# Both MLPs of a transform kernel as Strassen products, with weight combinations streamed from HBM

## The reference

```python
# attention without softmax, normalised per head
kv = einsum('bhsd,bhse->bhde', k, v); out = einsum('bhsd,bhde->bhse', q, kv)
x = out / sqrt(mean(out * out, -1) + 1e-6) * g_norm          # -> [B, S, D]
# first MLP: real part of a 2D Fourier transform, layer norm, MLP, residual
u = x + real(fft(fft(x, axis=1), axis=2))
x2 = u + relu(layer_norm(u) @ w_ch1) @ w_ch2                 # 512 -> 2048 -> 512
# second MLP: low-rank mixing over the tokens (rank 32), MLP, residual
u2 = x2 + transpose(transpose(x2) @ U @ V)
out = u2 + relu(u2 @ w_ch1b) @ w_ch2b
```

## Time and profile before

| what | value |
|---|---|
| median of 3 runs | 1966.59 us |
| the profiled execution, first to last instruction | 1964.7 us |
| granted TensorE clock, mean | 0.992 |
| TensorE busy | 1905.0 us, 97% |
| VectorE busy | 640.9 us, 33% |
| ScalarE busy | 359.1 us, 18% |
| GpSimd busy | 140.6 us, 7% |
| DMA | 94.96 MB, 48 GB/s over the span |

### The profile page before, as it was taken

The page is one execution under the profiler, slowest core; times in us unless marked ns, Lnnn a source line. Parts: engine busy times, 40 slices in busy tenths (PEclk is TensorE's granted clock), DMA queues, the critical chain, the costliest instruction groups (busy, mean ns, idle before and its releaser), DMA issues.

```text
span 1964.7 us, 24175 instructions
## 1 busy us (share of the span) xinstructions
PE 1905.0 (97%) x9764; PEld 1677.6 (85%) x9764; DVE 640.9 (33%) x1126; ACT 359.1 (18%) x784; POOL 140.6 (7%) x124
## 2 busy tenths in 40 slices
PE   5988799999999999999999999999999999999999
PEld 4777589999999999999988888888988888888988
DVE  4899962222222222222224321221222221221221
ACT  1333331111111111111123211211111111211111
POOL 1566530000000000000000000000000000000000
PEclk8999899999999999999999999999999999999999
DMA  8445230000000000000213100010000000000000
GB/s 298 163 157 168 95 120 33 1 32 32 31 1 32 32 0 32 32 32 0 80 58 107 65 33 17 17 34 7 27 33 1 33 33 17 17 17 1 17 17 16
DMA packets 23138, 94.96 MB, mean 48 GB/s; under 512 B 4833, under 2 KB 7265, under 8 KB 20130
## 3 DMA queue, kind: packets, MB, share of 16 engines
q1 hardware_dynamic: 23074, 94.01, 14.0%
HBM read 65.69 MB, written 28.31 MB: 48 GB/s over the span
## 4 chain that ended last, share of the span: by engine, by line
PE 88%; DVE 6%; DMA 1%; issue 1%; SPq 1%; POOL 1%; DVEq 0%; ACT 0%; POOLq 0%
PE bank L476 14%; PE bank L478 14%; PE bank L463 14%; PE bank L462 14%; PE bank L464 14%; PE bank L477 14%; PE bank L454 2%; DVE eo_sb L817 1%; DVE eo_sb L815 1%; DMA q_sb<-q_t 1%; PE bank L531 1%; POOL x_sb L1038 1%; DVE ss_sb L790 1%; SPq L209 1%; DVE x_sb L803 0%
## 5 line engine op out<-in xcount | busy, mean ns | idle before, releaser
L891 DVE SCALAR_TENSOR_TENSOR h_lo<-bank,h_hi 128x384 fp32r<-128x384 f32 x384 | 214.0, 557 | 1212.5 <-ACT h_hi L699 1212.5
L464 PE MATMUL bank<-at_hi,w_lo 128*128 128x384 f32 x1536 | 514.7, 335 | 2.1 <-issue 2.1
L462 PE MATMUL bank<-at_hi,w_hi 128*128 128x384 f32 x1536 | 515.0, 335 | 1.3 <-issue 1.3
L463 PE MATMUL bank<-at_lo,w_hi 128*128 128x384 f32 x1536 | 515.9, 336 | 0.0
L476 PE MATMUL bank<-w_hi,h_hi 128*128 128x512 f32 x1152 | 463.7, 403 | 0.0
L478 PE MATMUL bank<-w_hi,h_lo 128*128 128x512 f32 x1152 | 456.0, 396 | 0.0
L477 PE MATMUL bank<-w_lo,h_hi 128*128 128x512 f32 x1152 | 453.9, 394 | 0.0
L699 ACT ACTIVATE h_hi<-bank 128x384 fp32r<-128x384 f32 x384 | 189.2, 493 | 1369.2 <-PE bank L464 1369.2
L462 PEld LDWEIGHTS bank<-at_hi,w_hi 128*128 128x128 f32 x1536 | 288.4, 188 | 17.3 <-issue 2.1
L463 PEld LDWEIGHTS bank<-at_lo,w_hi 128*128 128x128 f32 x1536 | 288.1, 188 | 15.0
L464 PEld LDWEIGHTS bank<-at_hi,w_lo 128*128 128x128 f32 x1536 | 288.4, 188 | 2.7 <-issue 2.7
(11 more groups left out here) (84 smaller groups left out, 970.3 us busy)
## 6 DMA issues: line engine op xcount, KB each, us to landing
q_sb<-q_t SPq DMA_DIRECT2D x8, 1152.0 KB, 5.2
u_dram<-x_sb SPq DMA_DIRECT2D x24, 384.0 KB, 3.1
u_sb<-u_dram SPq DMA_DIRECT2D x12, 768.0 KB, 4.2
x_dram<-u_sb SPq DMA_DIRECT2D x12, 768.0 KB, 3.3
x_sb<-x_dram SPq DMA_DIRECT2D x12, 768.0 KB, 5.1
out<-u_sb SPq DMA_DIRECT2D x12, 768.0 KB, 3.3
k_sb<-k_main SPq DMA_DIRECT2D x7, 1024.0 KB, 5.2
v_sb<-v_main SPq DMA_DIRECT2D x7, 1024.0 KB, 7.6
```

The lines of the kernel that those rows point to most:

```text
L462: nc.tensor.matmul(ps[:, 0:TILE], w1_hi4[:, f, d, :], at_hi[:, d, :], start=(d == 0), stop=False)
L463: nc.tensor.matmul(ps[:, 0:TILE], w1_hi4[:, f, d, :], at_lo[:, d, :], start=False, stop=False)
L464: last = nc.tensor.matmul(ps[:, 0:TILE], w1_lo4[:, f, d, :], at_hi[:, d, :], start=False, stop=(d == ND - 1))
L891: nc.vector.scalar_tensor_tensor(h_lo[:, f % 2, :], hid_ps[f % 2][:, 0:TILE], 0.0, h_hi[:, f % 2, :].bitcast(F32), ALU.max, ALU.subtract). ...
```

## The change

**Strassen.** Both tiles of a pair are taken together: a group is 768 tokens of one MLP, and there are 12 groups (NG), six for each MLP (NS = 6). Each matrix product of a group is cut into 2 x 2 blocks and made as seven block products: activations `SIDE[i]` (a block, or the sum or difference of two) times a combination i of weight blocks. The seven results are added and subtracted into four blocks, partly in PSUM (products 2, 4 and 7 accumulate on each other in one bank pair, 5, 3 and 6 in another), partly by VectorE and ACT as they are read. Each product is still three matmuls of high and low parts. A step is (product i, block k) with 12 matmuls of 384 columns; a group has 28 up steps and 28 down steps. Both layers now give transposed outputs, so the first MLP's output is turned back by 144 transposes (`turn_out`), and the kernel's output is stored transposed.

```diff
-SPLIT_AT, GATHER_AT, TURN_AT, MIX_AT = 2, 3, 11, 12
+UP_STEPS = ([(1, k) for k in range(4)]
+            + [(i, 2 * h + j) for h in range(2) for i in (2, 4, 7) for j in range(2)]
+            + [(i, 2 * h + j) for h in range(2) for i in (5, 3, 6) for j in range(2)])
+DN_ORDER = (2, 5, 1, 4, 3, 7, 6)
+DN_STEPS = [(i, k) for i in DN_ORDER for k in range(4)]
+RING = 7
+ENT_RING = 5
+SIDE = {1: ("11", "22", 1), 2: ("11",), 3: ("12", "22", -1), 4: ("21", "11", -1), 5: ("22",), 6: ("11", "12", 1),
+        7: ("21", "22", 1)}
+OUT_AT = [1 + 4 * j for j in range(NCH)]
+POOL_KS = (3,)
...
+            def up_step(g, i, k):
+                e = UP_ENTRIES.index(i)
+                if k == 0:
+                    pe.wait_ge(lo_ready, entry(g, e))
+                w = weights_there(g, UP_SLOTS.index((i, k // 2)))
+                up_room(g, i, k)
...
+                for f in range(2):
+                    ps = pair[n][:, 512 * f:512 * f + TILE]
+                    for x in range(2):
...
+                        nc.tensor.matmul(ps, w_hi, hi[:, x, :], start=(fresh and x == 0), stop=False, skip_group_check=True)
+                        nc.tensor.matmul(ps, w_hi, lo[:, x, :], start=False, stop=False, skip_group_check=True)
+                        last = nc.tensor.matmul(ps, w_lo, hi[:, x, :], start=False, stop=(x == 1), skip_group_check=True)
```

```diff
+            def load_unit(unit):
+                name, n = unit[:2]
+                if n:
+                    sp.wait_ge(p_stored[name], 16 * n)
...
+            def store_unit(unit):
+                name, n, mlp, layer, f, x = unit
+                sp.wait_ge(p_lo[name], n + 1)
...
             next_kv(2)
-            sp.dma_start(w1_raw[:, :], w1a).then_inc(w_loaded[0][0], 16)
-            with sp.Fori(2, B - 1) as b:
+            load_unit(UNITS[1])
+            for b in range(2, B):
                 next_q(b)
-                next_kv(b + 1)
+                if b < B - 1:
+                    next_kv(b + 1)
+                store_unit(UNITS[b - 2])
+                load_unit(UNITS[b])
                 store_u(b - 2)
+            store_unit(UNITS[6])
+            load_unit(UNITS[8])
...
+            for q in range(NCH):
+                load_in(q)
...
+            store_unit(UNITS[7])
+            load_unit(UNITS[9])
+            store_unit(UNITS[8])
+            store_u(B - 2)
+            for n in range(RING):
+                load_w(n)
+            store_u(B - 1)
+            store_unit(UNITS[9])
...
+                        if t == 0:
+                            load_unit(UNITS[11])
+                            sp.wait_ge(last_stored, 16 * NT)
+                            load_unit(UNITS[10])
+                        if t in STORED_AT:
+                            store_unit(UNITS[10 + STORED_AT.index(t)])
...
             for g in range(NT):
                 weigh(0, g)
-            with pool.Fori(1, B) as b:
+            for b in range(1, B):
                 for g in range(NT):
                     weigh(b, g)
+                sum_unit(UNITS[b - 1])
                 for t in range(NT):
                     add_transform(b - 1, t)
```

More of the change, by code:

```diff
@@ L41, in build_program, with by_pool @@
+OUT_AT = [1 + 4 * j for j in range(NCH)]
+GATHER_AT = [4 + 4 * j for j in range(NCH)]
+MIX_AT = [28, 31, 34, 37, 41, 45]
+IN_AT = [30, 33, 36, 39, 43, 47]
+LN_AT = [8, 16, 38]
+STORED_AT = (4, 6, 12, 14, 20, 22)
+POOL_KS = (3,)
+def by_pool(i, k):
+    return k in POOL_KS
+def build_program(nc, k_main, k_rest, v_main, v_rest, q_t, g_norm, wr1a, wr2a, wr1b, wr2b, u_perm, v_perm,
+                  c_seq, s_seq, c_feat, s_feat, eye, u_dram, x2_dram, wc, out):
     F32 = mybir.dt.float32
@@ new lines, in build_program, with unit_blocks, raw_weights @@
+        UNIT_AT = {7 * (g - 1) + n: (g, 8 * n) for g in range(1, 6) for n in range(7) if 7 * (g - 1) + n < 32}
+        HALF_UNITS = {(g, n0): UNITS[16 + u] for u, (g, n0) in UNIT_AT.items()}
+        def unit_blocks(unit):
+            name, _, _, _, _, x = unit
+            _, raw, two = PB[name]
+            n = 1 if x is not None else 2
+            return [raw[:, n * i:n * (i + 1), 1, :] for i in range(7)], [two[:, i, :].rearrange("p (x c) -> p x c", x=n) for i in range(2)]
+        def raw_weights(unit, blk):
+            _, _, mlp, layer, f, x = unit
+            w = wr[mlp][layer][f]
+            return w[:, blk, :, :] if x is None else w[:, blk, x:x + 1, :]
@@ new lines, in gather @@
+            def gather(g, j):
+                n = NCH * g + j
+                tile, c = 2 * g + j // CH, j % CH
+                u = 3 * (tile % 3) + c
+                first, last = u == 0, u == 8
+                if n == 0:
+                    pe.wait_ge(up_split_lo, 1)
+                if first and n:
+                    pe.wait_ge(gt_lo_ready, tile // 3)
+                pe.wait_ge(x2_lo_ready, n + 1)
+                nc.tensor.matmul(gt_ps[0:64, :], up_hi[:, u, :], x2_hi[:, :], start=first, stop=False)
+                nc.tensor.matmul(gt_ps[0:64, :], up_lo[:, u, :], x2_hi[:, :], start=False, stop=False)
+                nc.tensor.matmul(gt_ps[0:64, :], up_hi[:, u, :], x2_lo[:, :], start=False, stop=last).then_inc(gathered, 1)
@@ L1052, in _, with raw_dn, add_first @@
+            def raw_dn(g, n):
+                i, k = DN_STEPS[n]
+                if len(SIDE[i]) > 1 and by_pool(i, k):
+                    raw(g, len(UP_ENTRIES) + n)
+            def add_first(g, block):
+                pool.wait_ge(dve_read, dve_count(g, "d1"))
+                nc.gpsimd.tensor_tensor(a_block(g, block), a_block(g, block), ch_block("22"), ALU.add).then_inc(v_ready, 1)
             for g in range(NT):
                 weigh(0, g)
-            with pool.Fori(1, B) as b:
+            for b in range(1, B):
@@ new lines, in _ @@
+            add_transform(B - 1, 0)
+            raw(0, 0)
+            add_transform(B - 1, 1)
+            add_transform(B - 1, 2)
+            sum_unit(UNITS[9])
+            raw(0, 2)
+            raw(0, 3)
+            for g in range(NG):
+                more = g < NG - 1
+                for t in range(NSTEP):
+                    if g == 0 and t + 2 in STORED_AT:
+                        sum_unit(UNITS[10 + STORED_AT.index(t + 2)])
+                    if t == 5:
+                        raw(g, 5)
+                    if t == 12:
+                        raw(g, 6)
+                    if 32 <= t < 52:
+                        raw_dn(g, t - 24)
+                    if g >= NS and t == 41:
+                        add_first(g, "11")
+                        add_first(g, "22")
+                    if more and t == 52:
+                        raw(g + 1, 0)
+                    if more and t == 54:
+                        raw(g + 1, 2)
+                    if more and t == 55:
+                        raw(g + 1, 3)
+                    if (g, t - 2) in HALF_UNITS:
+                        sum_unit(HALF_UNITS[g, t - 2])
```

1280 lines of the change are left out of this document (818 added, 462 removed), and 3 rows, old and new, of the table ACT_EV.

## The result

The changed kernel takes 2042.91 us, the median of 4 runs (2040.17 to 2048.87), beside 1965.83 (1964.09 to 1968.62) for the kernel before: the ratio is 1.0396, with a 95% interval of 1.0377 to 1.0416. It is slower; the forecast was 1956 us and its range ended at 2035. The profiled execution spans 2038.4 us at a mean granted clock of 0.941.

A forecast was written before the change was run, and what follows sets the result against it. VectorE was taken to bound the first phase, TensorE the MLPs. From 1964.7 us: matmuls -190, first phase +80, entrance +38, group 0 +40, groups 1 to 11 +22, giving 1954.7, so 1956 us as the median; range 1890 to 2035.

The forecast's parts named there:

- First phase: Attention and transform: a unit's store and four loads delay each batch's store, 13 us for six batches plus 2: +80 us.
- Entrance: Way into the MLPs: first up matmul 53 us after T, the loop's last row repair, instead of 15: +38 us.
- the data side hides behind the stores: Entrance: data ready at T + 41, hidden because the first weight slot, issued then behind stores, lands at T + 53.
- Group 0: Unit 10 waits behind seven weight loads and a store: step 6 idles 27, later units 8, clock 5; +40 us.
- Groups 1 to 11: VectorE's and GpSimd's work nearly fits TensorE's steps; 2 us of stalls a group: +22 us.
- rival C: Groups 1 to 4: DMA is the bound, 138 us a group at 307 GB/s; 48 us more, 2004 us; chance 0.12.
- second of its two signs: Rival C's signs, groups 1 to 4 alone: first, TensorE waiting for w_sb; second, VectorE waiting for units.
- Rival D: Narrow matmuls run at the 188 ns of a weight load, not 0.1733 us: 118 us more, 2074 us; chance 0.03.
- rival B: Second half of every group: VectorE is the bound, 8 us a group instead of 2: 2006 us; chance 0.23.
- A: First phase and entrance: weight units are mostly hidden, saving 55 and 23 us of the forecast: 1878 us; chance 0.15.

The follow-up runs named there:

- e7: Changed kernel with the six chunk loads at the entrance ahead of unit 6's store and unit 8's load in SyncE's queue: 2030.58 us.
- e3: Changed kernel without the second MLP's 32 half units (loads, sums, splits, stores); that MLP streams the first one's combinations instead: 1969.59 us.
- e2: Changed kernel with GpSimd's five sums of each half unit one step later, behind the inner block sum: 2012.37 us.
- e4: Changed kernel with all 20 inner block sums of a group on VectorE and none on GpSimd: 1992.6 us.
- e12: e8 with the half units' sums on GpSimd one step later, as in e2: 1924.63 us.
- e5: Changed kernel without weight streaming: only the first seven slots are loaded, and later steps use what lies in the ring: 1991.15 us.
- e13: Changed kernel with the ring of entries and all that lies behind it starting 32 bytes later: 2031.11 us, one run.
- e8: Changed kernel with the batch's store before the unit's, all inner sums on VectorE, group 0's queue reordered and entrance chunk loads ahead: 1925.35 us.

## Why the prediction was wrong

It said 1954.7 us for the span and the trace says 2038.4, 83.7 more. Along the path:

| term | forecast | trace | difference |
|---|---|---|---|
| last L1194 of the loop (L849 at 243.06 before) | +80 | 309.3: +66 | -14 |
| from there to the first up matmul (14.9 before) | +38 | 52.3: +37 | -1 |
| group 0 over 119.2 (672 x 0.1733 + 24 x 0.115) | +40 | 171.6: +52 | +12 |
| groups 1 to 11 over their share of the sum | +22 | +108 | +86 |

The last row: (1964.7 - 257.9) - 190 - 119.2 = 1397.6 without stalls, and the trace has 2038.4 - 533.2 = 1505.2. The first three terms together came to 155 where 158 was forecast, but partly by luck: 14 us too much in the first cancel 12 too little in the third.

**First phase: right in mechanism, 14 us too much.** Forecast 13 us a batch, measured 39.1 - 27.6 = 11.5; the store chain lies where it was put, L1155 waiting 9.5 us at most for `u_dram<-x_sb`. The first batch's 2 us more and the last's were not seen.

**Entrance: right.** The weight slot was forecast to be issued at T + 41 and went out at 349.92 - 309.3 = T + 40.6; the first matmul at T + 53, measured T + 52.3. That the data side hides behind the stores was too simple: in e7 the chunks came sooner, and with them the split and the store of unit 7, the slots and the first matmul, by 7 us.

**Group 0: right in place, 12 us short.** The store behind seven slots was to land at T + 78, it did at T + 74.5, and step 6 idles 23 us where 27 were forecast. The later units cost 15 and not 8 (7.1, 2.1 and 5.7 us at steps 14, 15 and 21). Some 64 starts at half clock cost 9 and not 5, the slower pace is 2, and smaller waits are the rest. TensorE's windows of the changed kernel show it at 1.2 GHz for 4 us behind an idle stretch and at 2.4 GHz behind that:

```profile
399.68:403.50 3.82, 3.82 (x12) 3.82 (x13) 2.52 (x2) 1.70 (x1) 2.06 (x2) 0.52 1.03 382
403.70:410.00 6.30, 6.30 (x37) 6.30 (x37) 3.55 (x8) 2.56 (x4) 0.00 (x0) 1.00 1.00 316
```

**Groups 1 to 11: the step that failed, "+22 us".** It should have been 108. Three things were measured, and with 2 us of half units in group 5 (e3, no more than that group varies) they make 101. The other 7 are not placed; the cost of GpSimd's inner sums in groups 1 to 4, which e3 keeps, may be among them:

- 68 us are the half units of groups 1 to 4 (e3). The prediction counted their DMA, and "norm, units, mixed chunks and add_first" as 3 to 5 us of VectorE's time a group, but never asked where `sum_unit` stands in GpSimd's order. It asked just this for SyncE in the first phase and in group 0. A sum waits up to 19.4 us for its loads with an inner sum behind it; e2 takes 30 us away with one step's delay, e4 36 us by moving that inner sum off the queue. These two are not shown to add: e12, which has both, is no better there than e4. What stays of the 68 with the inner sums moved is at least in part the unit's split in ACT's and VectorE's order (the rows of e4), which the prediction did not place either. e5 shows that 38 of the 68 come only with the stream: that is rival C's mechanism, priced at 48. It acts as the second of its two signs said, VectorE waiting for units (L1201 for ACT's L928: 23.9 us in groups 1 to 4), and not through late `w_sb`. C's rate did not set the changed kernel's 146 us a group, since e2 and e4 moved the same bytes in 137 to 139. It may set what remains above e3's 129.4: the same 170 MB in 518 us would need 328 GB/s, which no run held over these groups, though one short stretch of the changed kernel has 382 (the first row under group 0), more than the limit of about 358 that the prediction cites.
- 17 us are the pace, 7392 x (0.1767 - 0.1744). The forecast took the pace of the kernel before for the same shape, and read it from one round, 0.1733, which was 1.1 ns too low. Rival D had this term at 118 us; its mechanism, a pace set by the weight loads, is not shown, for the loads take 0.190 to 0.193 us in the changed kernel while the starts are 0.1767 apart.
- 14 us are GpSimd's inner sums in groups 6 to 11, where no half unit is (e4: 3.2, 3.1, 1.6, 1.6, 3.2, 1.3). That is rival B's mechanism, VectorE's full order, at the size of the forecast's own 2 us a group; but TensorE waits for the mixed chunk (L1351), and only 1.6 us for a low part.

A, B and D as priced did not come; C's 48 was the nearest to a part that did, the 68. The forecast, B and C were taken as alternatives, and what came was the forecast with a part of B and C and a slower pace; by that the time passed the end of the range.

**What stays open.** Of the pace's 2.3 ns the place of the ring explains 0.7 (e13); streaming, banks every 3, the distance of the low weights and that of the entries explain nothing. A bank kept for 12 matmuls, as before, was not tried. In e8 groups 1 to 4 are still 9 to 11 us each over e3's, and whether that is their split on ACT and VectorE or the rate of DMA, no run separates.
